# Fetching input weights one block earlier in a fused attention and gated-MLP kernel

## The reference

```python
# attention: q, k, v are (4, 8, 576, 64), scale = 1/8
out_d  = softmax(scale * mean4(q) @ mean4(k).T) @ mean4(v)      # tokens averaged in fours
scores = where(abs(i - j) < 4, scale * q @ k.T, -1e9)           # a narrow band
x = repeat(out_d, 4, axis=2) + softmax(scores) @ v              # -> (2304, 512)
# first MLP: w_gate, w_val (512, 1536), w_out (1536, 512)
x = (sigmoid(x @ w_gate) * (x @ w_val)) @ w_out
# second MLP: w_in (512, 2048), w_out (2048, 512)
h = x @ w_in
out = (h * sigmoid(1.702 * h)) @ w_out
```

## Time and profile before

| | |
|---|---|
| median of three runs | 1009.44 us (1008.92 to 1011.5) |
| the profiled execution, its own time | 1009.07 us |
| its span, first to last instruction | 1007.0 us |
| mean granted TensorE clock | 0.966 |
| TensorE matmuls busy | 925.3 us, 92% |
| POOL busy | 690.6 us, 69% |
| VectorE, ScalarE busy | 517.3 us (51%), 481.5 us (48%) |

### The profile page before, as it was taken

The page is one execution under the profiler, slowest core; times in us unless marked ns, Lnnn a source line. Parts: engine busy times, 40 slices in busy tenths (PEclk is TensorE's granted clock), DMA queues, the critical chain, the costliest instruction groups (busy, mean ns, idle before and its releaser), DMA issues.

```text
span 1007.0 us, 17570 instructions
## 1 busy us (share of the span) xinstructions
PE 925.3 (92%) x6566; PEld 853.6 (85%) x6566; DVE 517.3 (51%) x975; ACT 481.5 (48%) x964; POOL 690.6 (69%) x547
## 2 busy tenths in 40 slices
PE   8898999999999999878888999999788878887888
PEld 6777899999999999767777999999677767776777
DVE  6776445555555546444544454556445445534455
ACT  5777655554555544444434455444444343334432
POOL 5677779996799985566647599984775664335530
PEclk9999989999999999988999999999999999989999
DMA  9774112221212121211112113112111111231112
GB/s 312 222 218 115 57 43 66 82 84 64 64 63 80 68 63 44 82 43 42 42 66 81 63 63 126 64 63 84 43 43 53 74 42 43 62 126 43 42 47 79
DMA packets 26516, 79.59 MB, mean 79 GB/s; under 512 B 3136, under 2 KB 3136, under 8 KB 26432
## 3 DMA queue, kind: packets, MB, share of 16 engines
q1 hardware_dynamic: 26432, 78.48, 23.5%
HBM read 73.75 MB, written 4.72 MB: 78 GB/s over the span
## 4 chain that ended last, share of the span: by engine, by line
PE 73%; DMA 10%; POOL 7%; issue 4%; ACT 4%; DVE 2%; SPq 1%; ACTq 0%; DVEq 0%
PE o_ps L399 30%; DMA w_raw<-in_w_in_dram 9%; POOL w_sum L1304 6%; PE d_ps L409 6%; PE d_ps L411 5%; PE d_ps L412 5%; PE s_ps L409 5%; PE s_ps L412 4%; PE s_ps L411 4%; PE t_ps L411 2%; PE t_ps L412 2%; PE t_ps L409 2%; PE o_ps L372 1%; PE t_ps L357 1%; PE d_ps L332 1%
## 5 line engine op out<-in xcount | busy, mean ns | idle before, releaser
L1304 POOL TENSOR_TENSOR w_sum<-w_raw 128x256 f32<-128x256 f32 x120 | 88.6, 738 | 224.5 <-DMA w_raw<-in_w_in_dram 184.7
L1137 DVE TENSOR_TENSOR att<-o_ps,att 128x512 f32<-128x512 f32 (+1 forms) x246 | 153.1, 624 | 153.0 <-PE o_ps L399 152.6
L409 PE MATMUL d_ps<-xs_hi,w_hi 128*128 128x384 f32 x360 | 125.7, 349 | 36.9 <-ACT snap L760 35.2
L1329 POOL TENSOR_TENSOR w_lo<-w_sum,w_hi 128x1024 fp32r<-128x1024 f32 x60 | 143.9, 2398 | 2.2 <-ACT w_hi L705 2.2
L409 PE MATMUL s_ps<-xs_hi,w_hi 128*128 128x384 f32 x300 | 104.8, 349 | 29.2 <-ACT snap L760 29.0
L411 PE MATMUL d_ps<-xs_lo,w_hi 128*128 128x384 f32 x360 | 123.8, 344 | 0.0
L412 PE MATMUL d_ps<-xs_hi,w_lo 128*128 128x384 f32 x360 | 123.4, 343 | 0.0
L1340 POOL TENSOR_TENSOR v_lo<-v_raw,v_hi 128x1024 fp32r<-128x1024 f32 x42 | 100.5, 2392 | 31.8 <-ACT v_hi L709 31.6
L399 PE MATMUL o_ps<-v_hi,g_lo 128*128 128x512 f32 x288 | 120.1, 417 | 0.0
L399 PE MATMUL o_ps<-v_lo,g_hi 128*128 128x512 f32 x288 | 120.0, 417 | 0.0
L399 PE MATMUL o_ps<-v_hi,g_hi 128*128 128x512 f32 x288 | 118.2, 410 | 0.0
(11 more groups left out here) (120 smaller groups left out, 2090.9 us busy)
## 6 DMA issues: line engine op xcount, KB each, us to landing
v_raw<-in_w_out_dram SPq DMA_DIRECT2D x42, 512.0 KB, 3.5
w_raw<-in_w_gate_val_dram SPq DMA_DIRECT2D x36, 512.0 KB, 3.5
w_raw<-in_w_in_dram SPq DMA_DIRECT2D x24, 512.0 KB, 4.4
vw<-in_v_win_dram SPq DMA_DIRECT2D x32, 170.6 KB
vt<-in_v_tok_dram SPq DMA_DIRECT2D x16, 320.0 KB, 4.4
qk<-in_q_t_dram SPq DMA_DIRECT2D x16, 288.0 KB, 4.2
qk<-in_k_t_dram SPq DMA_DIRECT2D x16, 288.0 KB, 4.8
out_dram<-att SPq DMA_DIRECT2D x18, 256.0 KB, 4.6
```

Of the source, the lines that this page charges most:

```text
L409: pe.matmul(bank, wh[:, w, cols], xh[:, x, c, :], start=(start and c == 0), stop=False, skip_group_check=True)
L1137: vec.tensor_tensor(part, value, part, ALU.add).then_inc(y_added, 1)
L1304: x = gp.tensor_tensor(w_sum[b % 2][:, name, :], a, c, op)
L1329: gp.tensor_tensor(w_lo[b % 2][:, S1:S4 + 1, :], w_sum[b % 2][:, S1:S4 + 1, :], w_hi[b % 2][:, S1:S4 + 1, :], ALU.subtract).then_inc(ws_re ...
```

## The change

- `load_in(b)` waits for `wsum_ready` (POOL's sums of block b-1) beside `wa_ready`, and does nothing for a block past the last.
- SP's loop runs one block ahead where the groups are of MLP 2: in loop k it issues the block behind `FIRST[k+2]` (group k+3's in MLP 2), and the block behind `LAST[k+1]` if group k+1 is of MLP 1. Ahead of the loop, `load_in(2)` comes before `load_out(1)`.
- ScalarE: `round_in_sums` of the next first block leaves `next_first` and becomes `next_first_sums`, called after `hi11(k+1)`. In `from_two_to_two`, `round_x_step` comes after `snap_u3` and `sig22`.
- Transition: on ScalarE `snap_p1(0)` behind `drain_pooled(14)`, `round_in(1)` in unit 15, the first sigmoid (with its table load) after `snap_u2(0)`, `round_in_sums(2)` after `snap_u3(1)`; on VectorE `add_levels(14)` before `c11(0)`; on POOL the T3 rest one unit later, `sums_in_end(1)` after the last x, block 2's `low_in` before its sums, and `low_out(0)` behind all of block 2.

```diff
--- before.py
+++ after.py
@@ -233,8 +233,11 @@
 
             def load_in(b):
 
+                if b == len(BLOCKS):
+                    return
                 if b >= 1:
                     sp.wait_ge(wa_ready, b)
+                    sp.wait_ge(wsum_ready, b)
                 k, m = BLOCKS[b]
                 q, lay, p, g = GROUPS[k]
                 sp.dma_start(w_raw[:, :, :].rearrange("p a n -> p (a n)"), w_gate_val[g, m] if lay == 1 else w_in2[g]
@@ -275,16 +278,16 @@
                     load_out(0)
                 if i == 7:
                     load_in(1)
+            load_in(2)
             load_out(1)
-            load_in(2)
             load_in(3)
             for k in range(NG):
                 if k >= 1 and k + 1 < NG:
                     load_out(k + 1)
+                if k + 1 < NG and layer(k + 1) == 1:
+                    load_in(LAST[k + 1] + 1)
                 if k + 2 < NG:
-                    load_in(FIRST[k + 2])
-                    if layer(k + 2) == 1:
-                        load_in(LAST[k + 2])
+                    load_in(FIRST[k + 2] + 1)
                 for q in (2, 4):
                     if k == START[q + 1] + 1:
                         store(q)
@@ -810,6 +813,9 @@
 
                 if k + 2 < NG:
                     round_in(FIRST[k + 2])
+
+            def next_first_sums(k):
+                if k + 2 < NG:
                     round_in_sums(FIRST[k + 2])
 
             def from_one_to_one(k):
@@ -832,6 +838,7 @@
                 next_first(k)
                 snap_u2(w)
                 hi11(k + 1)
+                next_first_sums(k)
                 snap_u3(w)
 
             def from_one_to_two(k):
@@ -861,10 +869,11 @@
                 sig11(k + 1)
                 snap_u2(n)
                 hi11(k + 1)
+                next_first_sums(k)
                 round_out(k + 1)
-                round_x_step(k)
                 snap_u3(n)
                 sig22(k + 1)
+                round_x_step(k)
                 hi22(k + 1)
                 sig21(k + 1)
                 hi21(k + 1)
@@ -928,15 +938,15 @@
                     round_x_sum(0, T3, 4)
                 if i == 13:
                     round_x_sum(0, T4, 3)
-                if i == last - 1:
+                if i == last:
+                    round_in(1)
+                    snap_u2(0)
                     nc.scalar.activation(token[:, 1:2], token[:, 0:1], ACT.Sigmoid)
-                    snap_p1(0)
-                    round_in(1)
-                if i == last:
-                    snap_u2(0)
                     sig11(0)
                     snap_u3(0)
                 drain_pooled(i)
+                if i == last - 1:
+                    snap_p1(0)
                 if i + 2 < UNITS:
                     exps(i + 2)
                 if i + 1 < UNITS:
@@ -951,10 +961,10 @@
             sig12(0)
             snap_p1(1)
             round_in(2)
-            round_in_sums(2)
             snap_u2(1)
             hi11(0)
             snap_u3(1)
+            round_in_sums(2)
             for k in range(NG - 1):
                 if layer(k) == 1 and layer(k + 1) == 1:
                     from_one_to_one(k)
@@ -1228,8 +1238,8 @@
 
             normalise(UNITS - 2)
             inverse_pooled(UNITS - 1)
+            add_levels(UNITS - 2)
             c11(0)
-            add_levels(UNITS - 2)
             normalise(UNITS - 1)
             c22(0)
             add_levels(UNITS - 1)
@@ -1441,15 +1451,18 @@
                     low_x_sum(0, T2, 4)
                 if i == 13:
                     low_x_sum(0, T1, 5)
+                if i == 14:
                     low_x_sum(0, T3, 6)
-                if i == 14:
                     low_x_sum(0, T4, 7)
-                    sums_in_end(1)
             low_x(0, B22, quarter[1, 1], 3)
+            sums_in_end(1)
             low_in(1)
             low_in_sums(1)
+            low_in(2)
+            sums_in_begin(2)
+            sums_in_end(2)
+            low_in_sums(2)
             low_out(0)
-            split_in(2)
             for k in range(NG - 1):
                 if layer(k + 1) == 1:
                     split_in(LAST[k + 1])
```

## The result

The changed kernel takes 910.36 us (median of four runs, 909.52 to 911.52), against 1009.18 us for the kernel before beside it: a ratio of 0.902 (95% interval 0.900 to 0.904). The prediction was 909.3. The profiled execution has a span of 907.7 us, 99.3 less than before, and a mean clock of 0.996.

A forecast was written before the change was run, and what follows sets the result against it. TensorE was taken as full in the first MLP, but stalled and slow-clocked in the second by late `snap_u2`. Span 1007.0 - 96.7 (second MLP) - 3.5 (transition) = 906.8; plus 2.1 and 0.4, 909.3 us; range 904 to 935.

The forecast's parts named there:

- The chain fetch, sums, `round_in_sums`, `snap_u2`, `p7`: Second MLP: late weights delay POOL's sums, `round_in_sums`, then `snap_u2`, for which `p7` waits; 64.2 us of stalls, transition included.
- main term: Second MLP: 21 group periods, 425.15 us together, fall to 15.64 us each, saving 96.7 us.
- The split of that term: Second MLP: the 96.7 us are 60.8 of gaps, at most 2 of L766 waits, and 34 of slow clock.
- The walk through one group: Second MLP, one 15.64 us group: `snap_u2` ends at 5.2, 1.7 us spare; next sums end at 2.6; POOL works 13.3.
- The load's 5.8 us: Second MLP: time from SP's issue of a weight load until the weights are there and seen, 5.8 us.
- The first MLP: First MLP: `low_in_sums` 0.5 us later, some 0.35 us left before `p4`, lag absorbed at `low_out`; cost 0, bound 4.5 us.
- The transition: Between attention and first MLP: the 3.39 us stall gives way to a 2.3 us wait before `p6(2)`; gain 3.5 us.
- A new wait in each group: Rival, second MLP: POOL's late sums delay `snap_u3`, so `p4` waits; 930 us at 1 us a group; chance 0.11.
- A clock that stays low by itself: Rival, second MLP: gaps go but the 34 us of slow clock stay; 943 us; chance 0.04.
- The load is not the release: Rival: `snap_u2` stays late by something else and only the transition gains; 1003 to 1009 us; chance 0.06.
- The ring through `load_out`: Rival, second MLP: `load_out` behind a late `load_in` makes queues wait in a ring; 1016 us at 5.1 a group; chance 0.03.

The follow-up runs named there:

- ScalarE's order alone: Kernel before, with only `next_first_sums` moved behind `hi11` and `round_x_step` behind `sig22` on ScalarE; 939.50 us, ratio 0.932.
- SP alone: Kernel before, with only SP's main loop changed: second-MLP weights fetched one block earlier, with the added `wsum_ready` wait; 911.11 us, ratio 0.902.
- the late fetch: Changed kernel, with SP in the second MLP also waiting for `v_ready` before each weight load; 910.76 us, ratio 0.903.
- five extra copies: Changed kernel, with ScalarE repeating the `snap_u2` copy five times before telling TensorE, in each of 22 `from_two_to_two`; 936.55 us, ratio 0.928.
- nine extra copies: Changed kernel, with ScalarE repeating the `snap_u2` copy nine times before telling TensorE, in each of 22 `from_two_to_two`; 1007.82 us, ratio 0.9975.

## Why the prediction was right

- **The wait that mattered.** The chain fetch, sums, `round_in_sums`, `snap_u2`, `p7` held: the fetch alone takes it away (911.11), and the copy made late on purpose brings the old time back (1007.8). The prediction walked both edits of the loop as one and did not say which was needed; the fetch alone is enough.
- **The size of the main term.** 96.7 us were forecast from one group of the kernel before that had no weights to fetch. The 21 periods after are 328.39 us together, so 96.8 went and the term came out whole. This was the strongest part of the argument: the price was read, not composed.
- **The split of that term was off.** I called 34 us of it slow clock. Edges are in it too: the period from 839.10 to 857.77 has clock 1.00 and one gap of 2.76 us, and is 3.03 over 15.64, so 0.27 is edge. At that price the 23 stops (21 for `snap_u2`, 2 for `snap_u3`) cost 6 us, and some 28 are left for the slow clock (an estimate). Nor does each gap bring it: 5 of the 21 periods are at 1.00. It changed nothing in the sum, since the price was that of a whole period.
- **The walk through one group.** `snap_u2` at 5.2, sums ended at 2.7 and POOL's 2.5 us of room are as walked. The load's 5.8 us was mis-sized: 4.4 is usual in the kernel before, and 3.5 in the changed kernel, where it goes out alone. With 7 us of room it did not matter here; in the experiment with ScalarE's order alone it did.
- **The first MLP.** A lag of 0.5 us was forecast, with 0.35 us left for `snap_u3`, and its end at `low_out`. The profile has 0.55 and 0.30, and no wait. It is the narrowest place that I looked at in the loops of the changed kernel.
- **The transition.** Forecast 3.5 us, with a new gap of 2.3 us ahead of `p6(2)`. It gave 2.8 in the trace and 2.7 alone; the gap is 1.98. The clock did fall behind it, which I had left open (134.0 without, 136 with; 135.3 measured). So the term was 0.7 us too large. 96.8 and 2.8 are 99.6; the spans differ by 99.3, and the 0.3 are somewhere in the rest, the two longer groups of the first MLP among it.
- **The rivals.** A new wait in each group: none. A clock that stays low by itself: refuted, it is 1.00 in both windows of the changed kernel, and even 22 short gaps leave its mean at 0.998. The Trainium skill's rule for that rival (TensorE: Matmul & The Clock Gate, "A second HAM failure mode") is thus not borne out at gaps of 0.7 to 1.1 us once a group. The load is not the release: refuted by SP alone. The ring through `load_out`: `load_in` goes out 4.2 us into a period of 15.64, and at 11.6 in the experiment with the late fetch, still ahead of the group's end and with no loss.

## What to carry to other kernels

Look in the trace for the one iteration in which the suspected work is missing (the last one often has nothing to prefetch): its period is the price of the loop without the stall, gaps, edges and clock included. When a copy in an in-order queue is late, there are two ways out, to bring its predecessor's input earlier or to move the predecessor behind it; find out which one is enough, since the second may then add nothing, as here. A single buffer can be refilled as soon as its last reader is done: tie the fetch to that reader, not to the end of an iteration that happens to stand ahead in the queue.

## What the runs showed of the hardware

- A gap of 0.7 to 1.1 us of TensorE in each group left the granted clock at 1.00 (the kernels with five extra copies and with ScalarE's order alone). Gaps of 2.74 us brought a stretch at the lower level in 17 of 20 periods and none in 3 (nine extra copies); gaps of 2.6 to 4.1 us in 16 of 21 (the kernel before). The single gap of 2.00 us in the kernel with ScalarE's order alone was followed by it too: in the window from 835 to 838 us the clock was 0.67. So was the 1.98 us one ahead of `p6(2)`.
- A stop costs more than its row says, by some 0.3 us at full clock: 0.27 with a gap of 2.76 us (the kernel before), 0.24 to 0.32 with gaps of 0.8 to 1.05 us (the periods up to 518.45 of the kernel with ScalarE's order alone). A stop can also have no row at all: then the first matmul of a product takes 0.44 us instead of 0.33.
- The same 512 KB load took a median of 4.4 us from issue to landing when SP issued it straight behind another of 512 KB, and 3.5 us alone, first the kernel before, then the changed one:

```profile
w_raw<-in_w_in_dram SPq DMA_DIRECT2D x24, 512.0 KB, 4.4
```

```profile
w_raw<-in_w_in_dram SPq DMA_DIRECT2D x24, 512.0 KB, 3.5
```

- Three loads were slower until `round_in` began. In the kernel before, one took 5.83 us, with 1.44 us instead of 0.43 for SP's own issue, and one 5.84 us, with an issue of 0.43 but the six stores of a finished pass (256 KB each) issued right behind it. In the kernel with ScalarE's order alone, one took 6.94 us, with an issue of 1.51 and those stores behind it. What held the issues was not tried.
